# Expert stage of a fused attention and mixture-of-experts kernel: transposes move from TensorE to transposing DMAs on ScalarE's queue

## The chip, the cores and the metric

The kernel runs on one core of one Trainium2 chip. The metric is the device time of one execution in microseconds (us), the median of the runs shown. All rows come from one profiled execution of the same kernel.

## What is computed

The reference chains three stages. Only the last one, `_moe2_ref`, is touched here:

```
attn_out = _attn_ref(q, k, v, g_q, g_k)              # 4 x 12 heads, 448 x 64
x = attn_out as 1792 rows of 768
x = _moe_ref(x, w_gate, w_val, w_out)                # gated layer, 768 -> 1536 -> 768
# _moe2_ref: 8 experts, w1[e] is 768 x 1024, w2[e] is 1024 x 768
e_idx = argmax(x @ w_gate, axis=1)
gate_w = softmax(x @ w_gate) at e_idx
eom = sigmoid(x @ w_output_gate)
for e in range(8):
    mask = e_idx == e
    h = maximum(x[mask] @ w1[e], 0.0)
    ye = h @ w2[e]
    out[mask] = gate_w[mask, None] * eom[mask, e, None] * ye
```

Each row of x goes to one expert alone.

## The kernel before

Every matrix product of the fp32 data runs as three fp16 products: each operand is split into a high and a low fp16 part, and `PASSES` multiplies high by high, high by low and low by high. So a tile of 128 rows of x is 128 x 1536 fp16 (both parts), and a tile of the inner layer is 128 x 2048 fp16.

After the second stage the rows of x lie in DRAM as `y_parts`, high and low parts side by side. A routing table sorts them by expert into tiles of 128 rows, each tile of one expert. Tiles are numbered g from 0; an expert has one or more, and in this case there are 18. What each engine does for them is written out by hand as a function `tile(e, s, before, first)` for expert e, weight slot s, tile g = before + 1, and `over_experts` (line 381) calls it in loops whose bounds are read from the table. `first` marks an expert's first tile.

- **GpSimd** (`gather`, line 583) fetches the rows of tile g from `y_parts` into `x_rows`, two tiles ahead by its order but with one buffer only, so that it waits until the rows of the tile before have been transposed (`rows_turned`, line 601). `scatter` (line 606) stores finished rows.
- **TensorE** (`tile`, line 1533) does for tile g: `up` of half 0 (18 products of 128x512, line 1506), the transposes of the inner layer of the tile before (`turn_hidden`, 16 of 128x128, line 1515), `up` of half 1, the transposes of the gathered rows of tile g+1 (`turn_rows`, 12 of 128x128, line 1493), and `rows_down` of the tile before (48 products of 128x384, line 1528). Below, these are U0, U1 and D. `up` reads `x_t`, and `rows_down` reads `hid_t`; both are single buffers. Transposes land in PSUM.
- **VectorE** copies the transposed data from PSUM: `rows_out` (line 1229) into `x_t`, `turned_hidden` (line 1234) into `hid_t`. It also splits the inner layer (`hidden_split`, lines 1244 and 1246) and makes the low parts of the next expert's weights (`split_low`, line 1042).
- **ScalarE** (`tile`, line 838) takes the two halves of the inner layer out of PSUM with a Relu (line 848, hid0 and hid1 below), scales finished rows in `rows_done` (line 835, two instructions) once D has ended (`out_sum`), and makes the high parts of the next expert's weights (`split_high`, line 815). In an expert's first tile it makes three pieces before hid0, three between hid0 and hid1, and the last eight behind `rows_done`, so that these eight stand ahead of the next tile's hid0. Expert 1's first tile is an exception: there 14 pieces stand between hid0 and hid1 ("catch-up").
- **SyncE** loads the raw weights of the experts (line 512) into seven staging buffers, each as soon as `w_lo_ready` says that VectorE is done with it.

D of the tile before starts only when hid0 of the present tile is out, which also says that `rows_done` has emptied D's PSUM banks:

```
def tile(e, s, before, first):
    g = before + 1
    pe.wait_ge(x_t_ready, g + 1)
    up(e, s, g, 0, first)
    if not is_at(g, 0):
        turn_hidden(before, 0)
        turn_hidden(before, 1)
    up(e, s, g, 1, first)
    turn_rows(g + 1)
    if not is_at(g, 0):
        pe.wait_ge(hid_ready, 2 * g + 1)
```

Of the kernel before, what the change touches and what calls it, by code (L numbers as in the profile page):

```python
# [7 lines left out]
F16 = mybir.dt.float16  # L8
I32 = mybir.dt.int32
U32 = mybir.dt.uint32  # L10
ALU = mybir.AluOpType
# [45 lines left out]
def attention_moe_moe_kernel(nc, qk, v, v_last, g_qk, w_gate, w_val, w_out, w_out_t, router_w, out_gate_w,  # L57
# [19 lines left out]
    with ctx:  # L77
        def sem(name):
            return ctx.enter_context(nc.semaphore(name))
# [141 lines left out]
        hid = m2.take(128, F2, F32)  # L221
        hid_parts = m2.take(128, 2 * F2, F16).rearrange("p (l f) -> p l f", l=2)
        hid_t = m2.take(128, 2 * F2, F16).rearrange("p (b l c m) -> p b l c m", b=2, l=2, c=4)
# [104 lines left out]
        rows_turned = sem("rows_turned")  # L328
        x_t_ready = sem("x_t_ready")
# [4 lines left out]
        hid_turned = sem("hid_turned")  # L334
        hid_t_ready = sem("hid_t_ready")
        out_sum = sem("out_sum")
# [184 lines left out]
        def _(pool):  # L521
# [61 lines left out]
            def gather(g):  # L583

                if not isinstance(g, int):
                    read, turned, copied = pool.to_reg(16 * g), pool.to_reg(g), pool.to_reg(g + 1)
                    pool.wait_ge(route, ROUTE_DONE)
                    pool.wait_ge(gathered, read)
                else:
                    wait(pool, gathered, 16 * g)  # L590
                nc.gpsimd.tensor_copy(gather_idx, row_idx[:, bass.ds(g, 1)]).then_inc(gather_idx_ready, 1)
                if isinstance(g, int):
                    pool.wait_ge(gather_idx_ready, g + 1)
                    wait(pool, rows_turned, g)
# [56 lines left out]
        def _(act):  # L651
# [177 lines left out]

            def rows_done(g):  # L830

                act.wait_ge(out_sum, g + 1)
                act.wait_ge(scatter_idx_ready, g + 2)
                for b in range(2):
                    nc.scalar.activation(out_rows[:, b * HALF_DM:(b + 1) * HALF_DM], ps[:, 4 + b, 0:HALF_DM], ACT.Copy,  # L835
                                         scale=slot_w[:, bass.ds(g, 1)]).then_inc(out_ready, 1)

            def tile(e, s, before, first):
                g = before + 1
                more = first and not is_at(e, E - 1)  # L840
                if more and not is_at(g, 0):
                    act.wait_ge(hid_sum, 2 * g)
                    if not is_at(e, 1):
                        split_high(e + 1, 1 - s, range(0, KC // 2))
# [19 lines left out]
            rows_done(last_tile(act))  # L864

        @block.vector
        def _(dve):
# [354 lines left out]

            def rows_out(g):

                dve.wait_ge(rows_turned, g + 1)
                wait(dve, hid_sum, 2 * g)
                bank = 2 if is_at(g, 0) else 6
                for l in range(2):
                    last = nc.vector.tensor_copy(x_t[:, l].rearrange("p c m -> p (c m)"), ps[:, bank + l, :].bitcast(F16)[:, 0:DM])  # L1229
                last.then_inc(x_t_ready, 1)  # L1230
# [6 lines left out]
            rows_out(0)  # L1237
            split_low(0, 0, range(KC, PIECES))

            def hidden_split(g, b):  # L1240

                cols = slice(b * 512, (b + 1) * 512)
                dve.wait_ge(hid_ready, 2 * g + b + 1)
                nc.vector.tensor_copy(hid_parts[:, 0, cols], hid[:, cols]).then_inc(hid_hi_ready, 1)
                dve.wait_ge(hid_hi_ready, 2 * g + b + 1)
                nc.vector.tensor_tensor(hid_parts[:, 1, cols], hid[:, cols], hid_parts[:, 0, cols], ALU.subtract)\
                    .then_inc(hid_lo_ready, 1)

            def tile(e, s, before, first):
# [23 lines left out]
            over_experts(dve, tile)  # L1273
            last = last_tile(dve)
            turned_hidden(last, 0)
            turned_hidden(last, 1)

        @block.tensor
        def _(pe):
# [206 lines left out]

            def turn_rows(g):
                pe.wait_ge(gathered, 16 * g + 16)
                wait(pe, x_t_ready, g)
                bank = 2 if is_at(g, 0) else 6  # L1490
                for l in range(2):
                    for c in range(KC):
                        last = nc.tensor.transpose(ps[:, bank + l, :].bitcast(F16)[:, c * 128:(c + 1) * 128],  # L1493
                                                   x_rows[:, l * DM + c * 128:l * DM + (c + 1) * 128], ident)
                last.then_inc(rows_turned, 1)

            def up(e, s, g, b, first):


                if b == 1:  # L1500
                    wait(pe, hid_ready, 2 * g)
                for c in range(KC):
# [6 lines left out]

            def turn_hidden(g, b):  # L1510
                pe.wait_ge(hid_lo_ready, 2 * g + b + 1)
                for l in range(2):
                    for c in range(4):
                        at_c = b * 512 + c * 128
                        last = nc.tensor.transpose(ps[:, 2 + b, :].bitcast(F16)[:, (4 * l + c) * 128:(4 * l + c + 1) * 128],  # L1515
                                                   hid_parts[:, l, at_c:at_c + 128], ident)
                last.then_inc(hid_turned, 1)
# [31 lines left out]

            pe.wait_ge(route, ROUTE_DONE)  # L1550
            turn_rows(0)
# [47 lines left out]
```

## Time and profile before

| | |
|---|---|
| median of 3 runs | 1143.07 us (1142.74 to 1143.99) |
| the profiled execution's own time | 1139.88 us |
| its span | 1138.1 us |
| mean granted TensorE clock | 0.99 of full speed |
| TensorE busy | 1100.3 us, 97% of the span |
| VectorE busy | 594.7 us, 52% |
| ScalarE busy | 425.9 us, 37% |
| GpSimd busy | 256.5 us, 23% |
| first product of the expert stage | at 804.89 us of the span |

The span runs from the first to the last instruction of the profile. Busy time leaves out instructions that issue a DMA or wait. A share of DMA time is the mean over the core's 16 DMA engines. In a timeline each row is a run of like instructions with its start, its length and, in brackets, the idle time of that engine ahead of it with what ended it.

### The profile page before, as it was taken

The numbers are of one execution on the slowest core, as the hardware profiler recorded it, in microseconds if no ns is written. First come the engines' busy times: TensorE is split into PE (matmuls) and PEld (weight loads), VectorE is DVE, ScalarE is ACT, GpSimd is POOL, SyncE is SP. The second block draws the span as 40 slices with busy tenths as digits, with TensorE's granted clock in tenths as the row PEclk, the third lists the DMA queues.
The fourth block names the chain that finished last, engine by engine and source line by source line (L and its number), as shares of the span: only waits on it lengthen the run. The fifth ranks groups of instructions, "written<-read, shape, count | busy, mean of one in ns | idle before, by whom it ended". The sixth has DMA issues, their size and how long they took to land.

```text
span 1138.1 us, 17823 instructions
## 1 busy us (share of the span) xinstructions
PE 1100.3 (97%) x6617; PEld 573.3 (50%) x6618; DVE 594.7 (52%) x837; ACT 425.9 (37%) x631; POOL 256.5 (23%) x235
## 2 busy tenths in 40 slices
PE   7989999999999999999999999999898999999996
PEld 3434444444455555555555555556454555555554
DVE  7888888887433443333343300015656565556721
ACT  5768777777511111211111200001535253353510
POOL 4756767672200000000000000000211122112211
PEclk9999999999999999999999999999899999999999
DMA  5412222210121111111100501000848355366400
GB/s 144 122 49 62 61 65 58 66 25 17 60 67 56 56 55 55 55 55 55 55 28 1 195 28 41 28 32 23 296 163 319 118 211 206 108 217 225 142 20 18
DMA packets 71978, 104.11 MB, mean 91 GB/s; under 512 B 29310, under 2 KB 47870, under 8 KB 71920
## 3 DMA queue, kind: packets, MB, share of 16 engines
q1 hardware_dynamic: 63680, 89.84, 24.0%
q0 software_dynamic: 3120, 11.02, 2.7%
q10 hardware_dynamic: 5120, 2.48, 0.8%
q8 instruction: 36, 0.59, 0.2%
q14 instruction: 22, 0.18, 0.0%
HBM read 93.88 MB, written 13.76 MB: 95 GB/s over the span
## 4 chain that ended last, share of the span: by engine, by line
PE 87%; ACT 4%; DVE 4%; issue 2%; DMA 2%; ACTq 0%; POOL 0%; DVEq 0%; POOLq 0%; SPq 0%
PE ps L1434 29%; PE ps L1449 15%; PE ps L1528 12%; PE ps L1357 10%; PE ps L1506 7%; PE ps L1336 5%; PE ps L1316 2%; ACT arena L815 2%; DVE arena L1042 2%; PE ps L1348 2%; PE ps L1299 2%; PE ps L1338 1%; DMA arena<-in_moe_w 1%; PE ps L1515 1%; PE ps L1493 1%
## 5 line engine op out<-in xcount | busy, mean ns | idle before, releaser
L1434 PE MATMUL ps<-arena 128*128 128x448 f16 x1728 | 328.8, 352 | 0.0
L1434 PEld LDWEIGHTS ps<-arena 128*128 128x128 f16 x1728 | 168.1, 98 | 155.7
L1449 PE MATMUL ps<-arena 128*128 128x392 f16 (+1 forms) x1008 | 167.3, 329 | 2.4 <-DVE arena L1022 2.4
L1506 PE MATMUL ps<-arena 128*128 128x512 f16 x648 | 150.5, 388 | 5.6 <-DVE arena L1229 5.6
L1042 DVE SCALAR_TENSOR_TENSOR arena<-arena 128x768 f16<-128x768 f32 (+1 forms) x112 | 113.1, 1066 | 74.1 <-ACT arena L815 74.0
L1528 PE MATMUL ps<-arena 128*128 128x384 f16 x864 | 143.3, 326 | 4.0 <-DVE arena L1234 3.6
L1449 PEld LDWEIGHTS ps<-arena 128*128 (+1 forms) x1008 | 98.4, 98 | 70.4 <-DVE arena L1022 2.8
L1357 PE MATMUL ps<-arena 128*128 128x448 f32 x288 | 133.0, 573 | 0.0
L785 ACT ACTIVATE arena<-ps 128x448 f32<-128x448 f32 x48 | 26.1, 543 | 263.0 <-PE ps L1434 263.0
L1016 DVE SCALAR_TENSOR_TENSOR arena<-ps,arena 128x448 f32<-128x448 f32 x48 | 30.0, 624 | 176.0 <-PE ps L1434 96.1
L1528 PEld LDWEIGHTS ps<-arena 128*128 128x128 f16 x864 | 83.5, 98 | 58.6 <-issue 2.5
L940 DVE TENSOR_REDUCE arena<-ps 112x2 f16<-112x896 f32 x96 | 99.2, 1076 | 18.6 <-PE ps L1316 18.5
L815 ACT ACTIVATE arena<-arena 128x768 f16<-128x768 f32 (+1 forms) x112 | 97.5, 929 | 27.6 <-DMA arena<-in_moe_w 23.7
L1506 PEld LDWEIGHTS ps<-arena 128*128 128x128 f16 x648 | 63.7, 100 | 80.1 <-DVE arena L1229 6.4
L712 ACT ACTIVATE arena<-ps,arena 128x896 f32<-128x896 f32 x72 | 72.5, 1007 | 33.3 <-PE ps L1338 33.3
L960 DVE RECIPROCAL arena<-arena 128x448 f32<-128x448 f32 x24 | 70.8, 2951 | 10.3 <-ACT arena L730 10.3
L1336 PE MATMUL ps<-arena 64*128 64x448 f16 (+1 forms) x576 | 72.0, 356 | 3.0 <-ACT arena L712 1.7
L620 POOL MEMSET arena<- 128x1536 f16 x1 | 1.4, 1377 | 324.1 <-PE ps L1434 324.1
L835 ACT ACTIVATE arena<-ps,arena 128x384 f32<-128x384 f32 x36 | 18.9, 576 | 141.4 <-PE ps L1528 141.4
L1357 PEld LDWEIGHTS ps<-arena 128*128 128x128 f32 x288 | 47.6, 191 | 45.5 <-issue 45.5
L802 ACT ACTIVATE arena<-ps 128x768 f16<-128x768 f32 x14 | 11.3, 810 | 144.0 <-PE ps L1449 144.0
L1076 DVE TENSOR_SCALAR arena<-ps 128x16 f32 (+1 forms) x12 | 2.1, 171 | 119.9 <-ACT arena L802 119.9
(170 smaller groups left out, 1078.7 us busy)
## 6 DMA issues: line engine op xcount, KB each, us to landing
arena<-in_moe_w SPq DMA_DIRECT2D x48, 512.0 KB, 6.3
arena<-in_moe_w SPq DMA_DIRECT2D x64, 384.0 KB, 3.9
arena<-in_qk SPq DMA_DIRECT2D x23, 448.0 KB, 3.5
y_parts<-arena SPq DMA_DIRECT2D x16, 384.0 KB, 2.3
arena<-in_v SPq DMA_DIRECT2D x48, 96.0 KB, 2.6
arena<-in_moe_w_out SPq DMA_DIRECT2D x12, 384.0 KB, 5.5
arena<-in_w_out_t SPq DMA_DIRECT2D x11, 384.0 KB, 3.1
arena<-in_moe_w_gate SPq DMA_DIRECT2D x10, 384.0 KB, 4.2
```

The source lines that it names most:

```text
L712: nc.scalar.activation(probs[n % 2][:, :, i - 1], ps_pair(SCORE_SLOT, 128), ACT.Exp, bias=lift[:, 1:2])\
L815: nc.scalar.activation(hi, raw_rows(e, p), ACT.Copy, scale=S_OP).then_inc(w_hi_ready, 1)
L940: nc.vector.tensor_reduce(neg_max[n % 2][:, :, j], ps_pair(max_slot(n, j)), AX_X, ALU.max, negate=True)\
L960: nc.vector.reciprocal(sums_inv[n % 2], sums[n % 2]).then_inc(sums_inv_ready, 1)
L1016: nc.vector.scalar_tensor_tensor(gated[b % 2], ps[:, 2 * (b % 2) + 1, 0:S], 1.0 / S_OP, gate[b % 2], ALU.mult, ALU.mult).then_inc(gated_re ...
L1042: nc.vector.scalar_tensor_tensor(lo, raw_rows(e, p), S_OP, hi, ALU.mult, ALU.subtract).then_inc(w_lo_ready, 1)
L1336: nc.tensor.matmul(outs[h], qk_t[n % 3][rows, 1, kl, ks], qk_t[n % 3][rows, 0, ql], start=(kl + ql == 0), stop=False)
L1357: last = nc.tensor.matmul(ps[:, 6 + h, SQ], v_ones[n % 3][:, c, h * D:h * D + 2 * D], probs[n % 2][:, h, c], start=False, stop=(c == KCH - 1))
L1434: last = nc.tensor.matmul(ps[:, 2 * (b % 2) + g, 0:S], up_w[s][:, g, c, wl], xt[:, b * KC + c, xl], start=(c == 0 and wl + xl == 0), stop= ...
L1449: last = nc.tensor.matmul(ps[:, 4 + 2 * s + h, 0:cols], gt[:, f, gl, bass.ds(t * 128, 128)], wo[:, f, wl, h, 0:cols], start=(f == 0 and gl ...
L1506: last = nc.tensor.matmul(ps[:, b, :], x_t[:, xl, c], w1_s[s][:, c, wl, b * 512:(b + 1) * 512], start=(c == 0 and xl + wl == 0), stop=(c = ...
L1528: last = nc.tensor.matmul(ps[:, 4 + h, 0:HALF_DM], hid_t[:, b, hl, c], w2_s[s][:, k, wl, h * HALF_DM:(h + 1) * HALF_DM], start=(k == 0 and ...
```

## The change

`turn_rows` and `turn_hidden` leave TensorE, `rows_out` and `turned_hidden` leave VectorE. In their place ScalarE issues one transposing DMA for the rows of a tile (`x_rows` to `x_t`, 128 x 1536 fp16) and two for the halves of the inner layer (`hid_parts` to `hid_t`, 128 x 1024 fp16 each). Tile 0's rows are still transposed by TensorE. `hid_parts` changes its layout, so that a half lies in one piece, and VectorE's `hidden_split` waits until the half of the tile before has been transposed.

ScalarE issues the rows' DMA of tile g+1 behind hid1 of tile g. It issues the two DMAs of tile g's inner layer behind its wait for the end of D of tile g-1 (`out_sum`), since D reads `hid_t`, and ahead of the two copies of `rows_done`. For tile 0, which has no D ahead of it, they come directly behind the rows' DMA. The last tile's come in `rows_done` of the last call of `tile`. On ScalarE the names of the numbered lines are: 836 the rows' DMA, 844 the inner layer's, 858 the copies of `rows_done`, 871 the Relu, 816 `split_high`.

```diff
@@ gpsimd, gather
-                    pool.wait_ge(rows_turned, turned)
+                    pool.wait_ge(x_turned, turned)
@@ scalar
+            def turn_rows(g):
+
+                read = 16 * g + 16 if isinstance(g, int) else act.to_reg(16 * g + 16)
+                act.wait_ge(route, ROUTE_DONE)
+                act.wait_ge(gathered, read)
+                act.dma_start_transpose(x_t.rearrange("p l c m -> p (l c) m"), x_rows).then_inc(x_turned, 16)
+
+            def turn_hidden(g):
+
+                for b in range(2):
+                    split = 2 * g + b + 1 if isinstance(g, int) else act.to_reg(2 * g + b + 1)
+                    act.wait_ge(route, ROUTE_DONE)
+                    act.wait_ge(hid_lo_ready, split)
+                    act.dma_start_transpose(hid_t[:, b].rearrange("p l c m -> p (l c) m"), hid_parts[:, b].rearrange("p l f -> p (l f)"))\
+                        .then_inc(hid_turned[b], 16)
+
+            def rows_done(g, more_follow):
+
+                if more_follow:
+                    summed = act.to_reg(g + 1)
+                    act.wait_ge(route, ROUTE_DONE)
+                    act.wait_ge(out_sum, summed)
+                    turn_hidden(g + 1)
+                else:
+                    act.wait_ge(out_sum, g + 1)
...
+                turn_rows(g + 1)
                 if is_at(g, 0):
+                    turn_hidden(0)
                     split_high(e + 1, 1 - s, range(KC))
                 else:
-                    rows_done(before)
+                    rows_done(before, True)
@@ vector
-            def turned_hidden(g, b):
-                dve.wait_ge(hid_turned, 2 * g + b + 1)
-                nc.vector.tensor_copy(hid_t[:, b].rearrange("p l c m -> p (l c m)"), ps[:, 2 + b, :].bitcast(F16))\
-                    .then_inc(hid_t_ready, 1)
...
+                wait(dve, hid_turned[b], 16 * g)
+                nc.vector.tensor_copy(hid_parts[:, b, 0], hid[:, cols]).then_inc(hid_hi_ready, 1)
...
-                if not is_at(g, 0):
-                    turned_hidden(before, 0)
-                    turned_hidden(before, 1)
...
-                rows_out(g + 1)
@@ tensor
             def rows_down(e, s, g):
...
-                    pe.wait_ge(hid_t_ready, 2 * g + b + 1)
+                    pe.wait_ge(hid_turned[b], 16 * g + 16)
...
-                pe.wait_ge(x_t_ready, g + 1)
+                if is_at(g, 0):
+                    pe.wait_ge(first_x_ready, 1)
+                else:
+                    pe.wait_ge(x_turned, 16 * g)
                 up(e, s, g, 0, first)
-                if not is_at(g, 0):
-                    turn_hidden(before, 0)
-                    turn_hidden(before, 1)
                 up(e, s, g, 1, first)
-                turn_rows(g + 1)
...
-            turn_hidden(last, 0)
-            turn_hidden(last, 1)
```

TensorE before, one tile of the last expert (1506 is `up`, 1515 and 1493 the two kinds of transposes, 1528 `rows_down`):

```order
L1506 MATMUL ps<-arena 128x512 x18
L1511 ISA
L1515 MATMUL ps<-arena 128x128 x8
L1511 REGISTER_ALU
L1515 MATMUL ps<-arena 128x128 x8
L413 ISA
L1506 MATMUL ps<-arena 128x512 x18
L1488 ISA
L1493 MATMUL ps<-arena 128x128 x12
L1544 REGISTER_ALU
L1528 MATMUL ps<-arena 128x384 x48
```

TensorE with the change, the same tile (`up` is now line 1515, and 1523 is the wait for the turned inner layer):

```order
L413 ISA
L1515 MATMUL ps<-arena 128x512 x36
L1543 REGISTER_ALU
L1523 ISA
L1528 MATMUL ps<-arena 128x384 x48
```

The 28 transposes of a tile are gone, both halves of `up` run on without a break, and D of the tile before follows them at once.

ScalarE before, from hid1 of an expert's first tile to hid0 of the next tile, with what each instruction waits for:

```order
L848 ACTIVATE arena<-ps 128x512 [waits hid_lo_ready,hid_sum]
L833 REGISTER_ALU [waits out_sum]
L835 ISA [waits scatter_idx_ready]
L835 ACTIVATE arena<-ps,arena 128x384 x2
L815 ACTIVATE arena<-arena 128x768 [waits stage_loaded6]
L815 ACTIVATE arena<-arena 128x768 [waits stage_loaded0]
```

ScalarE with the change, the same place:

```order
L871 ACTIVATE arena<-ps 128x512 [waits hid_lo_ready,hid_sum]
L833 ISA
L836 DMA_TRANSPOSE arena<-arena 128x12x128 [waits gathered,route]
L844 DMA_TRANSPOSE arena<-arena 128x8x128 [waits route,hid_lo_ready,out_sum]
L844 DMA_TRANSPOSE arena<-arena 128x8x128 [waits hid_lo_ready,route]
L858 ISA [waits scatter_idx_ready]
L858 ACTIVATE arena<-ps,arena 128x384 x2
L816 ACTIVATE arena<-arena 128x768 [waits stage_loaded6]
L816 ACTIVATE arena<-arena 128x768 [waits stage_loaded0]
```

Three DMA issues now stand in ScalarE's order: one between hid1 and the wait for D's end, two between that wait and everything that follows it, the eight pieces of the weights and the next tile's hid0 among it.

## Rows read from the trace of the kernel before

**Rows 1.** The page's chain of work that ended last, by engine.

```profile
PE 87%; ACT 4%; DVE 4%; issue 2%; DMA 2%; ACTq 0%; POOL 0%; DVEq 0%; POOLq 0%; SPq 0%
```

**Rows 2.** Timeline of TensorE, tiles 4 to 7: start us, length us, what, idle before.

```profile
877.02 4.05 PE L1506 MATMUL ps<-arena 128*128 128x512 f16 x18
880.90 1.06 PE L1515 MATMUL ps<-arena 128*128 128x128 f16 x16
881.79 4.05 PE L1506 MATMUL ps<-arena 128*128 128x512 f16 x18
885.68 0.83 PE L1493 MATMUL ps<-arena 128*128 128x128 f16 x12
886.35 7.96 PE L1528 MATMUL ps<-arena 128*128 128x384 f16 x48
894.15 4.05 PE L1506 MATMUL ps<-arena 128*128 128x512 f16 x18
...
929.06 4.05 PE L1506 MATMUL ps<-arena 128*128 128x512 f16 x18
```

**Rows 3.** Timeline of ScalarE, tiles 5 and 6 (first and second of expert 2).

```profile
894.53 1.05 ACT L835 ACTIVATE arena<-ps,arena 128x384 f32<-128x384 f32 x2 [8.05 <-PE ps L1528]
896.23 2.95 ACT L815 ACTIVATE arena<-arena 128x1024 f16<-128x1024 f32 x3 [0.66 <-issue]
899.09 0.58 ACT L848 ACTIVATE arena<-ps 128x512 f32<-128x512 f32 x1
899.57 2.94 ACT L815 ACTIVATE arena<-arena 128x1024 f16<-128x1024 f32 x3
...
912.60 5.24 ACT L815 ACTIVATE arena<-arena 128x768 f16<-128x768 f32 x7
918.04 0.84 ACT L815 ACTIVATE arena<-arena 128x768 f16<-128x768 f32 x1 [0.21 <-DMA arena<-in_moe_w]
918.79 0.58 ACT L848 ACTIVATE arena<-ps 128x512 f32<-128x512 f32 x1
```

**Rows 4.** Timeline of TensorE, the first tiles of the stage.

```profile
816.56 0.84 PE L1493 MATMUL ps<-arena 128*128 128x128 f16 x12 [2.04 <-DMA arena<-y_parts,arena]
818.52 5.75 PE L1506 MATMUL ps<-arena 128*128 128x512 f16 x18 [1.12 <-DVE arena L1229]
...
837.35 4.05 PE L1506 MATMUL ps<-arena 128*128 128x512 f16 x18
...
857.00 5.56 PE L1506 MATMUL ps<-arena 128*128 128x512 f16 x18 [2.36 <-DVE arena L1229]
```

**Rows 5.** Timeline of ScalarE, catch-up of expert 1: its first piece and the hid1 behind its last.

```profile
841.93 5.23 ACT L815 ACTIVATE arena<-arena 128x768 f16<-128x768 f32 x7
...
858.57 0.58 ACT L848 ACTIVATE arena<-ps 128x512 f32<-128x512 f32 x1
```

**Rows 6.** Timeline of TensorE, the last tile.

```profile
1120.09 1.06 PE L1515 MATMUL ps<-arena 128*128 128x128 f16 x16
1121.57 7.97 PE L1528 MATMUL ps<-arena 128*128 128x384 f16 x48 [0.43 <-ACT arena L835]
```

**Rows 7.** Timeline of ScalarE in the first stage: DMAs issued from its own queue.

```profile
27.12 0.39 ACTq L676 DMA_DIRECT2D arena<-in_moe_w_gate  x1
...
29.15 2.01 ACTq L676 DMA_DIRECT2D arena<-in_moe_w_val  x1
```

**Rows 8.** DMA issues: engine, count, KB each, median us from issue to landing.

```profile
arena<-in_moe_w SPq DMA_DIRECT2D x48, 512.0 KB, 6.3
...
y_parts<-arena SPq DMA_DIRECT2D x16, 384.0 KB, 2.3
...
arena<-in_moe_w_gate ACTq DMA_DIRECT2D x1, 24.0 KB, 3.1
```

**Rows 9.** Landing of the gathers (line 602, 384 KB each), least, median and most.

```profile
DMA to landing us min/median/max: 2.2/5.8/7.8
```

**Rows 10.** DMA queue of ScalarE: packets, MB, share of the 16 engines' span.

```profile
q10 hardware_dynamic: 5120, 2.48, 0.8%
```

**Rows 11.** Windows of 4 us in tiles 5 and 6: engines' busy time, clock, DMA share, GB/s.

```profile
904.00:908.00 4.00, 4.00 (x26) 2.42 (x25) 3.97 (x7) 0.00 (x0) 2.06 (x2) 1.00 0.57 175
...
920.00:924.00 4.00, 3.52 (x30) 2.29 (x29) 3.97 (x8) 0.60 (x1) 1.25 (x2) 1.00 1.00 404
```

More of the change, by code:

```diff
@@ L221, in attention_moe_moe_kernel @@
         hid = m2.take(128, F2, F32)
-        hid_parts = m2.take(128, 2 * F2, F16).rearrange("p (l f) -> p l f", l=2)
+        hid_parts = m2.take(128, 2 * F2, F16).rearrange("p (b l f) -> p b l f", b=2, l=2)
         hid_t = m2.take(128, 2 * F2, F16).rearrange("p (b l c m) -> p b l c m", b=2, l=2, c=4)
@@ L328, in attention_moe_moe_kernel @@
         rows_turned = sem("rows_turned")
-        x_t_ready = sem("x_t_ready")
+        first_x_ready = sem("first_x_ready")
+        x_turned = sem("x_turned")
         hid_sum = sem("hid_sum")
@@ L333, in attention_moe_moe_kernel @@
         hid_lo_ready = sem("hid_lo_ready")
-        hid_turned = sem("hid_turned")
-        hid_t_ready = sem("hid_t_ready")
+        hid_turned = [sem(f"hid_turned{b}") for b in range(2)]
         out_sum = sem("out_sum")
@@ L585, in gather @@
                 if not isinstance(g, int):
-                    read, turned, copied = pool.to_reg(16 * g), pool.to_reg(g), pool.to_reg(g + 1)
+                    read, turned, copied = pool.to_reg(16 * g), pool.to_reg(16 * g - 16), pool.to_reg(g + 1)
                     pool.wait_ge(route, ROUTE_DONE)
@@ L593, in gather @@
                     pool.wait_ge(gather_idx_ready, g + 1)
-                    wait(pool, rows_turned, g)
+                    wait(pool, rows_turned, min(g, 1))
+                    wait(pool, x_turned, 16 * (g - 1))
                     if is_at(g, 0):
@@ L828, in _ @@
             split_high(0, 0, range(KC, PIECES))
-            def rows_done(g):
-                act.wait_ge(out_sum, g + 1)
+            def turn_rows(g):
[18 more added lines that the diff above has]
+                    act.wait_ge(out_sum, g + 1)
                 act.wait_ge(scatter_idx_ready, g + 2)
@@ L863, in _ @@
             over_experts(act, tile)
-            rows_done(last_tile(act))
+            rows_done(last_tile(act), False)
         @block.vector
@@ L1221, in _, with first_rows_out @@
             y_low(TT - 1, 1)
[L1223 to L1227, printed above, removed]
+            def first_rows_out():
+                dve.wait_ge(rows_turned, 1)
                 for l in range(2):
-                    last = nc.vector.tensor_copy(x_t[:, l].rearrange("p c m -> p (c m)"), ps[:, bank + l, :].bitcast(F16)[:, 0:DM])
-                last.then_inc(x_t_ready, 1)
-            def turned_hidden(g, b):
-                dve.wait_ge(hid_turned, 2 * g + b + 1)
-                nc.vector.tensor_copy(hid_t[:, b].rearrange("p l c m -> p (l c m)"), ps[:, 2 + b, :].bitcast(F16))\
-                    .then_inc(hid_t_ready, 1)
-            rows_out(0)
+                    last = nc.vector.tensor_copy(x_t[:, l].rearrange("p c m -> p (c m)"), ps[:, 2 + l, :].bitcast(F16)[:, 0:DM])
+                last.then_inc(first_x_ready, 1)
+            first_rows_out()
             split_low(0, 0, range(KC, PIECES))
@@ L1243, in hidden_split @@
                 dve.wait_ge(hid_ready, 2 * g + b + 1)
-                nc.vector.tensor_copy(hid_parts[:, 0, cols], hid[:, cols]).then_inc(hid_hi_ready, 1)
+                wait(dve, hid_turned[b], 16 * g)
+                nc.vector.tensor_copy(hid_parts[:, b, 0], hid[:, cols]).then_inc(hid_hi_ready, 1)
                 dve.wait_ge(hid_hi_ready, 2 * g + b + 1)
-                nc.vector.tensor_tensor(hid_parts[:, 1, cols], hid[:, cols], hid_parts[:, 0, cols], ALU.subtract)\
+                nc.vector.tensor_tensor(hid_parts[:, b, 1], hid[:, cols], hid_parts[:, b, 0], ALU.subtract)\
                     .then_inc(hid_lo_ready, 1)
@@ L1273, in _ @@
             over_experts(dve, tile)
-            last = last_tile(dve)
-            turned_hidden(last, 0)
-            turned_hidden(last, 1)
         @block.tensor
@@ L1484, in _, with turn_first_rows @@
             down(TT - 1, 1, range(4, FC))
[L1487 to L1490, printed above, removed]
+            def turn_first_rows():
+                pe.wait_ge(gathered, 16)
                 for l in range(2):
                     for c in range(KC):
-                        last = nc.tensor.transpose(ps[:, bank + l, :].bitcast(F16)[:, c * 128:(c + 1) * 128],
+                        last = nc.tensor.transpose(ps[:, 2 + l, :].bitcast(F16)[:, c * 128:(c + 1) * 128],
                                                    x_rows[:, l * DM + c * 128:l * DM + (c + 1) * 128], ident)
@@ L1497, in up @@
             def up(e, s, g, b, first):
-                if b == 1:
-                    wait(pe, hid_ready, 2 * g)
+                wait(pe, hid_ready, 2 * g + b - 1)
                 for c in range(KC):
@@ L1508, in up @@
                 last.then_inc(hid_sum, 1)
[L1510 to L1517, printed above, removed]
             def rows_down(e, s, g):
@@ L1550, in _ @@
             pe.wait_ge(route, ROUTE_DONE)
-            turn_rows(0)
+            turn_first_rows()
             over_experts(pe, tile)
             last = last_tile(pe)
-            turn_hidden(last, 0)
-            turn_hidden(last, 1)
             pe.wait_ge(out_ready, 2 * last)
```

## The prediction

> **What bounds the kernel now.** I read the chain of waits by engine first: 87% of it is TensorE [rows 1], so time leaves this kernel only where TensorE stops working or waiting. Then TensorE's timeline in the stage touched. A tile is five pieces on end without a gap: U0, transposes of the inner layer, U1, transposes of the rows, D. From 877.02 to 894.15 that is 17.13 us [rows 2]. The differences of the starts give U0 3.88, inner transposes 0.89, U1 3.89, row transposes 0.67, D 7.80. Products alone are 15.57, so the two kinds of transposes cost 1.56 us a tile. Third, ScalarE's timeline, because the change puts its DMAs there. In an expert's first tile and at the head of its second ScalarE is nearly full: the row copies, 3 + 3 pieces of weights around hid0, later eight more [rows 3]. Where these eight stand ahead of hid0, hid0 starts at 918.79 and D could start at 919.4; TensorE was ready for D only at 920.6. ScalarE has 1.2 us to spare there, and the change takes TensorE's work away and adds to ScalarE's.
>
> **What goes.** At most 1.56 us x 18 tiles = 28.1 us of TensorE, plus short waits of D for VectorE's copy. VectorE's copies vanish too, which is worth nothing by itself.
>
> **What comes: two unknown prices.** The trace has no transposing DMA. (a) The time for which ScalarE's queue is held by one issue, C. A plain issue with 768 pieces took 0.39 us when the queue was empty and 2.01 us as the fourth in a row [rows 7]. A transposing DMA has 1024 or 1536 pieces of 256 bytes if it is read so, and the two for the inner layer follow each other. I take 2.0 for each, the row with the queue filled, and keep 0.4 as the lower end. (b) The time L from its issue to its landing. A plain store of 384 KB out of the same memory takes 2.3 us, weight loads with several in flight take 6.3 [rows 8], gathers of 384 KB take 2.2 to 7.8, median 5.8 [rows 9]. The DMA share in tiles 5 and 6 is 0.57 to 1.00 [rows 11], so I take 7.0 for the rows (issue included) and 5.5 for half an inner layer.
>
> The Trainium skill, "Advanced Engine Details and Errata", section "X-Bar Transpose (TRN2)", holds that a transposing DMA is as fast as a plain one; no row here shows one. By that, L would lie near the 2.3 us of the plain store where the DMA engines are free, and the sum would be that of rival A.
>
> **The sum.** Let T be the end of a D, on which ScalarE waits.
>
> *Plain tiles* (4, 9, 16, 17). hid1 is done 7.77 + 0.6 after T, so the rows land at T + 8.4 + 7.0 = 15.4, just before D of the tile ends at 15.57. The inner layer lands at T + 7.5, before the next D at T + 7.77. So 1.56 us saved each: 4 x -1.56 = -6.2.
>
> *First and second tile of experts 2 to 6* (5 pairs; one takes 929.06 - 894.15 = 34.91 now [rows 2]). First tile: two issues 4.0, copies 1.05, gap and three pieces 3.60 (895.58 to 899.18), hid0 0.49 [rows 3], together 9.14. D waits for it: it runs from T + 9.14 to 16.94, where it could have begun at 7.77. Then three pieces (2.84) and hid1 (0.6) end at 12.6, and the rows land at 19.6. TensorE stands idle from 16.94 to 19.6. Second tile: ScalarE starts at 16.94: 4.0, copies 1.05, gap 0.1, eight pieces with their wait 6.3 (912.60 to 918.88), hid0 0.5, so D may start at 28.9; TensorE is ready at 19.6 + 7.77 = 27.4. D ends at 36.7. The pair takes 36.7 for 34.9: +1.8, five times +9.0. What is late next is the weights' pieces behind the two issues, but they have the rest of the tile.
>
> *The start.* Tile 1's rows land in x_rows at 816.56, and U0 starts at 818.52 behind TensorE's 0.84 and VectorE's copy [rows 4]. There is no D to cover the DMA, so U0 starts at 816.56 + 7.0 = 823.6. U0 5.6 and U1 3.9 follow, D ends at 840.9, where it was 837.35 [rows 4]: +3.6. ScalarE then issues two more (4.0) and copies, so hid0 of tile 2 ends at 846.5. Here the catch-up starts, which ran from 841.93 to 858.57 [rows 5], partly waiting for loads. Before, VectorE copied tile 3's rows in the middle of it, and U0 of tile 3 could start at 857.00. Now ScalarE issues that DMA behind the whole catch-up: starts 4.6 later, some of its waits for loads vanish, I put its end at 861 and hid1's at 861.6. The rows land at 868.6, U0 starts 11.6 us later than before. With 5.5 + 3.9 for the two halves and 7.8 for D, tile 4 starts at 885.8 against 877.02: +8.8.
>
> *The end.* The last tile's inner layer may only be transposed when the D before it has ended. Now 1.48 us lie between that and the last D (1120.09 to 1121.57 [rows 6]); with the change it is 5.5: +4.0. The second half's landing is covered by the first half of D.
>
> Together 8.8 + 9.0 - 6.2 + 4.0 = +15.6. The profiled execution took 1139.88, so 1155.5; the median of the runs is 3.2 above that execution, so 1158.7, say **1159 us**. With the bounds left open around it this case reaches from 1146 to 1210.
>
> **Rival A: the DMA is cheap.** C = 0.5, L = 4.0. First tile: hid0 at T + 6.1, D not delayed, rows landed at 13.6: 15.57. Second: D may start at 9.0, ends at 16.8. A pair is 32.3 instead of 34.9: five times -2.6 = -13.0. Plain -6.2. Start: rows at 820.6, end of D at 837.9, hid1 of the catch-up at 859.6, rows of tile 3 at 863.6, tile 4 starts +3.8. End: +1.5. Sum -13.9: 1126 for the execution, **1129** as a median. For it speak the 2.3 us of the plain store; against it the pieces of 256 bytes, and the bursts of weight loads that fall on just these tiles. The point that decides is C: every us on it adds 2 us to each hid0 that stands behind the two issues. At C = 1.2 and L = 6 the sum is about nil.
>
> **Rival B: the DMA engines (or the issue itself) become the bound.** Each tile turns 12 + 8 + 8 blocks of 128x128. ScalarE's queue moved 5120 packets in 0.8% of 16 engines' span, 28 ns each [rows 10]. If only the reads count, 3584 pieces of 256 bytes on 16 engines are 6.4 us a tile, hidden. If every 32-byte run that is written costs as much, that is 28,672 pieces or 51 us a tile, and 18 x (51 - 17) = +610. That small pieces are dear is to be seen in 24 KB that took 3.1 us, more than 384 KB in long ones [rows 8]. A price of 18 us a tile, near the geometric middle, and 7 us of weight loads (6.3 MB an expert at 404 GB/s [rows 11], 8 experts on 18 tiles) make 25 us instead of 17.1: **about 1285**. That the two patterns spread over fewer than 16 engines would look the same.
>
> The Trainium skill, "VectorE: DVE Perf Modes", section "The three transpose paths", gives 1309 ns for a 128x128 fp16-sized block by DMA and 390 ns by TensorE. As an estimate from that page, 28 blocks one after the other would be 36.7 us, and the time near 1490. TensorE's own block here goes by faster than the page's figure: 0.89 us for 16, that is 56 ns [rows 2].
>
> **How the numbers follow.** The forecast (issue and landing of middling price) 0.47, rival A 0.29, rival B 0.24. A measurement of this kernel can tell about 0.2% (2.3 us) from no change. Faster than 1140.8: 0.26, nearly all of A. Within: 0.07, the seam between A and the forecast. Slower: 0.67. The range reaches from 1122 (A with L at 2.3 to 3) to 1340, which takes in the nearer half of B; about 0.05 lie below and 0.13 above.
>
> **What the next profile would show.** ScalarE's queue rows for the transposing DMAs, with their length (2.0?) and landing (7 and 5.5?). TensorE's tile in plain stretches: 15.6 us, with no row of 128x128 products but tile 0's. Idle time ahead of U0, released by the rows' DMA: some 5 us at tile 1, most at tile 3, 2.7 in second tiles. Idle time ahead of D released by ScalarE's copies or Relu in the pairs, 1.4 to 1.5 us each. About 5.5 us ahead of the last D. I am wrong if the landing of the rows is under 4 us and the issue under 0.6 (then A), or if TensorE waits in plain tiles too, by 8 us or more (then B).

## The result and the profile after

The changed kernel takes 1186.58 us (median of 4, 1182.73 to 1193.4) against 1142.9 us of the kernel before beside it: a ratio of 1.039, with a 95% interval of 1.034 to 1.044. It is slower, as forecast, but by 43.7 us where 15.6 were forecast. Its profiled execution has a span of 1183.5 us, 45.4 more than before.

The page of the changed kernel, engines' busy time, then queues, then the chain of waits by engine:

```profile
PE 1090.2 (92%) x6113; PEld 547.8 (46%) x6114; DVE 557.1 (47%) x765; ACT 424.8 (36%) x631; POOL 252.1 (21%) x235
...
q1 hardware_dynamic: 63680, 89.84, 24.6%
q10 hardware_dynamic: 71360, 19.01, 10.0%
...
PE 76%; DMA 11%; ACT 3%; ACTq 3%; issue 3%; DVE 2%; POOL 1%; POOLq 0%; SPq 0%; DVEq 0%
```

TensorE is busy for 10.1 us less and idle for 55.5 us more. The chain that was TensorE's for 87% [rows 1] is TensorE's for 76%, and 11% of it is DMA. ScalarE's queue moved 66,240 packets more [rows 10]. Its share rose by 9.2 points of the time of the 16 DMA engines (16 x 1183.5 us), so 26 ns a packet, and 6.05 us of all 16 engines for each of the 18 tiles.

Who waited for whom on TensorE from 800 us on, total, times, longest:

```profile
PE ps L1515 <- DMA arena<-arena: 51.2, 12, 17.6
PE ps L1528 <- ACT arena L871: 5.0, 4, 3.0
PE ps L1528 <- ACT arena L858: 4.1, 1, 4.1
PE ps L1528 <- DVE arena L1067: 3.5, 3, 2.5
```

Here 1515 is `up` and 1528 is D. Most of the idle time stands ahead of U0, and the rows' DMA ends it. TensorE's timeline shows where (U0 and U1 are one row of 36 products now):

```profile
825.28 10.81 PE L1515 MATMUL ps<-arena 128*128 128x512 f16 x36 [9.77 <-DMA arena<-arena]
...
877.05 10.52 PE L1515 MATMUL ps<-arena 128*128 128x512 f16 x36 [17.59 <-DMA arena<-arena]
...
897.83 7.94 PE L1515 MATMUL ps<-arena 128*128 128x512 f16 x36 [2.45 <-DMA arena<-arena]
...
913.40 7.93 PE L1515 MATMUL ps<-arena 128*128 128x512 f16 x36
922.05 7.97 PE L1528 MATMUL ps<-arena 128*128 128x384 f16 x48 [0.71 <-ACT arena L871]
935.06 10.53 PE L1515 MATMUL ps<-arena 128*128 128x512 f16 x36 [5.03 <-DMA arena<-arena]
946.12 7.97 PE L1528 MATMUL ps<-arena 128*128 128x384 f16 x48 [0.53 <-ACT arena L871]
957.40 9.62 PE L1515 MATMUL ps<-arena 128*128 128x512 f16 x36 [3.31 <-DMA arena<-arena]
...
1122.39 7.97 PE L1528 MATMUL ps<-arena 128*128 128x384 f16 x48 [2.97 <-ACT arena L871]
1130.20 7.93 PE L1515 MATMUL ps<-arena 128*128 128x512 f16 x36
1137.97 7.96 PE L1528 MATMUL ps<-arena 128*128 128x384 f16 x48
1145.77 7.93 PE L1515 MATMUL ps<-arena 128*128 128x512 f16 x36
...
1165.56 9.65 PE L1528 MATMUL ps<-arena 128*128 128x384 f16 x48 [4.05 <-ACT arena L858]
```

Tile 4 starts at 897.83 instead of 877.02 [rows 2]; 1.0 us of that lies ahead of the stage. The pair of tiles 5 and 6 takes 957.40 - 913.40 = 44.0 us instead of 34.9. Tiles 16 and 17, beside which no weights are loaded, run as the forecast's plain tiles do: 15.57 us from one U0 to the next. A row of 36 products takes 7.93 us, but 9.6 to 10.8 behind most of the longer waits. From tile 1 on there are twelve waits of 2 us or more, and behind ten of them the next row of products is 1.7 to 2.9 us longer. Behind two it is not: 2.45 us ahead of tile 4, and 2.97 us ahead of the D at 1122.39.

ScalarE's queue, in its timeline: a DMA's issue with its length, first beside weight loads, then in the quiet tiles (the second row is the copies of `rows_done`).

```profile
866.60 9.62 ACTq L844 DMA_TRANSPOSE arena<-arena  x2
879.14 1.05 ACT L858 ACTIVATE arena<-ps,arena 128x384 f32<-128x384 f32 x2 [13.51 <-POOL arena L612]
...
921.52 2.29 ACTq L836 DMA_TRANSPOSE arena<-arena  x1
...
930.42 7.67 ACTq L844 DMA_TRANSPOSE arena<-arena  x2
...
1138.32 1.29 ACTq L836 DMA_TRANSPOSE arena<-arena  x1
1146.02 2.64 ACTq L844 DMA_TRANSPOSE arena<-arena  x2
```

And the 18 DMAs of the rows (line 836), least, median and most:

```profile
L836 ACTq DMA_TRANSPOSE arena<-arena x18: 1290/1924/6012, 818.5 to 1153.9; - x18
...
DMA to landing us min/median/max: 3.7/9.6/13.4
```

The DMA at 1138.32, which sees no weight loads, holds the queue for 1.29 us and lands in 3.7. The median one lands in 9.6, the worst in 13.4. In the five pairs nine of the ten land in 8.1 to 13.4 us.

Late rows hold up more than TensorE. GpSimd fetches the next rows only when these have been transposed, and behind that it writes the scatter index (line 612) for which ScalarE's copies wait. At tile 3 the two issues ended at 876.22, the rows landed at 876.93, and the copies began only at 879.14.

Two windows of the changed kernel, while loads and a transposing DMA were both in flight, with the columns of [rows 11]:

```profile
925.40:929.40 4.00, 4.00 (x27) 2.39 (x26) 3.17 (x4) 0.00 (x0) 0.00 (x0) 1.00 1.29 102
...
933.40:937.40 4.00, 2.34 (x6) 0.89 (x7) 0.00 (x0) 0.00 (x0) 1.25 (x2) 0.51 1.03 327
```

In the first the DMA engines are taken all the time (packets on one engine overlap, so the share passes 1.00) and move 102 GB/s, where loads alone move 404 in such a window [rows 11]. In the second, which holds the end of a wait of 5.03 us and the first products behind it, TensorE's granted clock is 0.51, its lower level of 1.2 GHz.

### The profile page after: what moved, and what is told of

Same layout as the page of the kernel before. It is cut to its first block, busy times and chain, and to the rows that moved or that the text cites. A ratio compares the mean times of both kernels' runs of the same rounds, so it can differ in the third digit from the quotient of the medians.

```text
span 1183.5 us, 16771 instructions
## 1 busy us (share of the span) xinstructions
PE 1090.2 (92%) x6113; PEld 547.8 (46%) x6114; DVE 557.1 (47%) x765; ACT 424.8 (36%) x631; POOL 252.1 (21%) x235
## 4 chain that ended last, share of the span: by engine, by line
PE 76%; DMA 11%; ACT 3%; ACTq 3%; issue 3%; DVE 2%; POOL 1%; POOLq 0%; SPq 0%; DVEq 0%
PE ps L1446 28%; PE ps L1461 14%; PE ps L1369 10%; DMA arena<-arena 8%; PE ps L1515 6%; PE ps L1528 6%; PE ps L1348 4%; PE ps L1328 2%; DMA arena<-in_moe_w 2%; ACTq L844 2%; PE ps L1311 2%; PE ps L1360 1%; PE ps L1350 1%; ACT arena L816 1%; DVE arena L1067 1%
## 5 line engine op out<-in xcount | busy, mean ns | idle before, releaser
L1446 PEld LDWEIGHTS ps<-arena 128*128 128x128 f16 x1728 | 168.1, 98 | 155.7
L1515 PE MATMUL ps<-arena 128*128 128x512 f16 x648 | 161.0, 413 | 53.4 <-DMA arena<-arena 51.2
L1528 PE MATMUL ps<-arena 128*128 128x384 f16 x864 | 146.8, 331 | 12.6 <-ACT arena L871 5.0
L1515 PEld LDWEIGHTS ps<-arena 128*128 128x128 f16 x648 | 66.9, 105 | 144.6 <-issue 80.0
L1528 PEld LDWEIGHTS ps<-arena 128*128 128x128 f16 x864 | 84.8, 99 | 74.9 <-issue 16.1
L816 ACT ACTIVATE arena<-arena 128x768 f16<-128x768 f32 (+1 forms) x112 | 97.0, 928 | 33.4 <-DMA arena<-in_moe_w 19.8
L603 POOL DMA_INDIRECT arena<-y_parts,arena x20 | 21.8, 1090 | 220.3 <-DMA arena<-arena 219.3
```

The costliest lines, as they stand in the source:

```text
L816: nc.scalar.activation(hi, raw_rows(e, p), ACT.Copy, scale=S_OP).then_inc(w_hi_ready, 1)
L1446: last = nc.tensor.matmul(ps[:, 2 * (b % 2) + g, 0:S], up_w[s][:, g, c, wl], xt[:, b * KC + c, xl], start=(c == 0 and wl + xl == 0), stop= ...
L1515: last = nc.tensor.matmul(ps[:, b, :], x_t[:, xl, c], w1_s[s][:, c, wl, b * 512:(b + 1) * 512], start=(c == 0 and xl + wl == 0), stop=(c = ...
L1528: last = nc.tensor.matmul(ps[:, 4 + h, 0:HALF_DM], hid_t[:, b, hl, c], w2_s[s][:, k, wl, h * HALF_DM:(h + 1) * HALF_DM], start=(k == 0 and ...
```

## The experiments

After the result there were three suspects: the landing beside weight loads (Q), the hold of ScalarE's queue by the issues (I) and its order (O), and TensorE's clock behind waits (K). Of each edit the lines that matter are shown; `...` marks a gap.

**One kind of transposes each.** rows_only keeps `turn_hidden` on TensorE and `turned_hidden` on VectorE; hid_only keeps `turn_rows` and `rows_out` there.

```diff
--- rows_only, from the changed kernel
-                    turn_hidden(g + 1)
...
--- hid_only, from the changed kernel
-                turn_rows(g + 1)
...
```

> Only the gathered rows are transposed by DMA; the inner layer goes through TensorE and VectorE as before. Theory Q (a transposing DMA lands late while weight loads share the DMA engines, and the rows' DMA has only one D, 7.8 us, to hide behind): nearly the whole loss is here. 40 to 51 us of TensorE waiting ahead of U0 and some 8 us of slower clock, less 18 x 0.67 saved: 1170 to 1185 us. Theory I (each issue holds ScalarE's queue for 1.3 to 6 us, and the pieces of weights and hid0 behind it come late): the rows' issue stands where ScalarE waits for D anyway, so little is lost but at tiles 1 and 3: 1145 to 1155 us.

> Only the inner layer is transposed by DMA; the rows go through TensorE and VectorE as before. Theory Q: its landing has U0 and U1 to hide behind, and the first half may be late by up to 1 us: saved 18 x 0.89 = 16 us, lost 2.5 us at the end and about 1 us a pair in ScalarE's delay: 1130 to 1140 us. Theory I: 36 of the 54 issues are here, 2.6 to 9.6 us a tile ahead of the row copies, the eight pieces and hid0: D waits for hid0 in every pair: 1155 to 1175 us.

Measured: rows_only 1163.91 us, ratio 1.017 (1.014 to 1.019); hid_only 1157.82 us, ratio 1.012 (1.010 to 1.014). Neither theory has both. The rows cost 20 us, below Q's range and above I's; the inner layer costs 14 us, in I's range. Waits on TensorE in rows_only, where 1515 is `up` and 1537 D, with the landing of its 18 DMAs:

```profile
PE ps L1515 <- DMA arena<-arena: 34.3, 7, 17.3
PE ps L1537 <- DVE arena L1247: 8.9, 6, 2.8
...
DMA to landing us min/median/max: 3.6/6.0/12.6
```

and in hid_only, where 1523 is D, with the landing of its 36 DMAs:

```profile
PE ps L1523 <- ACT arena L862: 11.0, 3, 4.7
PE ps L1523 <- DVE arena L1057: 7.9, 3, 2.7
...
DMA to landing us min/median/max: 3.1/3.3/8.4
```

So the two halves of the change lose in different ways. The rows' DMA lands late, and U0 waits for it. The inner layer's lands in 3.3 us and is in time, but D waits for ScalarE and VectorE, which come late behind the issue.

The two losses add to 34 us, not 44, and the traces show where the rest arises. From the stage's first product to the start of tile 4 rows_only is 21.0 us behind the kernel before, hid_only 6.1, the changed kernel 19.8. From there to the start of the last D it is 4.1, 8.3 and 23.2. So behind tile 4 the two halves are dearer together. In rows_only the rows that are issued in the pairs' first tiles land in 5.2 to 7.2 us, where the changed kernel has 8.1 to 13.4. In tile 5 one sees why: in rows_only the DMA's packets fall into a gap of the loads (926 to 929 us, 45 of the loads' packets in three us), while in the changed kernel it is issued at 921.52, just as the loads start, and its packets run among theirs. For the other pairs this was not looked at packet by packet.

**The order at the catch-up.**

```diff
-                        if is_at(e, 1):
-                            split_high(e, s, range(KC, PIECES))
-                            split_high(e + 1, 1 - s, range(0, KC // 2))
...
                 turn_rows(g + 1)
+                if more and is_at(e, 1):
+                    split_high(e, s, range(KC, PIECES))
+                    split_high(e + 1, 1 - s, range(0, KC))
```

> The changed kernel, but in expert 1's first tile ScalarE takes hid1 and issues the rows' DMA ahead of the 14 pieces of the catch-up instead of behind them. The changed kernel waits 17.6 us ahead of tile 3 for these rows. If the order on ScalarE is the cause of that wait (Q and I both say so), it shrinks to the 5 us that other tiles wait or to what the late weights leave, 1172 to 1180 us. If the loads of the weights bound this stretch anyway, the wait moves to the next D or U0: 1184 to 1188 us.

Measured: 1183.09 us (1172.53 to 1189.12), ratio 1.036 (1.032 to 1.039), not to be told from the changed kernel's 1.039, and in neither expected range. The profiled execution is the fastest of the four, 1172.53 us; the other three took 1183 to 1189. Waits of its TensorE:

```profile
PE ps L1515 <- DMA arena<-arena: 24.6, 9, 11.6
PE ps L1528 <- ACT arena L871: 18.2, 4, 14.2
```

The 17.6 us ahead of U0 of tile 3 are gone, and 14.2 us stand ahead of the D behind it instead, where the pieces now delay hid0. The order sets the place of that wait. What moving it gains can't be told: nothing by the median, while the one profiled execution lies inside the range expected for a gain.

**The clock.**

```diff
                 g = before + 1
+                if not is_at(g, 0) and not is_at(e, E - 1):
+                    keep_busy()                            # 10 products of 128x512 into an unused bank
```

> The changed kernel with ten more products of 128x512 (2.2 us at full clock, results unused) ahead of each tile's wait for its rows, in experts 0 to 6. Theory K (a part of the loss is that TensorE's clock falls to its lower level after a wait and U0 then runs 1.7 to 2.6 us longer): where the wait is over 2.2 us the products cost nothing and U0 and U1 go back from 9.6 to 7.9 us: 8 to 9 waits, 10 to 15 us less, but about 2.2 us more at each of the 4 tiles that wait for nothing: 1172 to 1182 us. If the clock plays no part: 1186 to 1200 us.

Measured: 1177.84 us, ratio 1.030 (1.027 to 1.033), 8.7 us below the changed kernel, although ten products were added to each of 15 tiles, tiles that had no wait among them. Three rows of its timeline, the added products (line 1535) and the `up` behind them:

```profile
952.59 2.32 PE L1535 MATMUL ps<-arena 128*128 128x512 f16 x10
956.80 7.94 PE L1515 MATMUL ps<-arena 128*128 128x512 f16 x36 [1.89 <-DMA arena<-arena]
...
1049.05 7.94 PE L1515 MATMUL ps<-arena 128*128 128x512 f16 x36 [0.45 <-DMA arena<-arena]
```

These are tiles 7 and 12, which took 9.62 and 9.63 us in the changed kernel behind waits of 3.31 and 2.23. From tile 1 on `up` takes 138.0 us in all instead of 151.4, so K holds as a part of the loss. At tiles 1 and 3 the wait outlasts the ten products (9.09 and 14.45 us more), and there U0 and U1 still take 9.57 and 9.32 us.

**Fewer bytes of weights, and more.**

```diff
--- light_before, light_after
-                    sp.dma_start(raw_rows(e, p), piece(e, s, p)[0]).then_inc(stage_loaded[p % STAGES], 16)
+                    few = (F2 if p < KC else DM) // (1 if isinstance(e, int) else 4)
+                    sp.dma_start(raw_rows(e, p)[:, 0:few], piece(e, s, p)[0][:, 0:few]).then_inc(stage_loaded[p % STAGES], 16)
--- endload_before, endload_after
+            sp.wait_ge(w_lo_ready, PIECES * E)
+            for k in range(24):
+                wait(sp, more_loaded[k % STAGES], 16 * (k // STAGES))
+                sp.dma_start(stage[k % STAGES], w1_d[k % 8, 0]).then_inc(more_loaded[k % STAGES], 16)
```

> The kernel before, with only the first quarter of the columns of each weight piece loaded for experts 2 to 7 (the same number of loads, a quarter of the bytes; the stale rest is split as if it were weights). All theories: before waits for loads only around tiles 2 to 4, so 1138 to 1143 us.

> The changed kernel with the same quarter loads. Theory Q (traffic: transposing DMAs land late because weight loads are on the DMA engines with them): landing of the rows goes back to about 3.7 us in nearly every tile, the waits ahead of U0 vanish from tile 5 on, and what is left is the start (10 to 20 us more than before up to tile 4), about nil in the pairs and 4 to 6 us at the end, less 1.56 us in plain tiles: 1150 to 1162 us. Theory O (order: ScalarE's issues and the catch-up are late by themselves, whatever the loads): 1175 to 1185 us as with full loads.

> The kernel before, with 24 more loads of 512 KB, not used by anything, once the last weights are split, so that the last two tiles, which saw no loads, now run beside them. Before has nothing there but gathers and scatters on the DMA engines, which it can wait for: within 2 us of before, 1141 to 1146 us.

> The changed kernel with the same 24 loads behind its last weights. In the changed kernel tiles 16 and 17 wait for nothing and their DMAs land in 3.7 and 3.3 us. Theory Q: beside full loads the rows land in 10 to 13 us, so that U0 of tile 17 waits 3 to 6 us, the inner layer's first half comes late, and the end waits 8 to 12 us instead of 4: 1195 to 1210 us. Theory O: 1186 to 1190 us.

Measured: light_before 1140.42 us, ratio 0.997 (0.995 to 0.998); light_after 1149.27 us, ratio 1.005 (1.003 to 1.006). The change costs 8.9 us beside quarter loads and 43.7 beside full ones. The expectation's range for light_after, 1150 to 1162, was just missed on the low side. Its waits (1516 is `up`, 1529 D) and the landing of its rows' DMAs:

```profile
PE ps L1529 <- ACT arena L872: 18.2, 11, 3.1
PE ps L1516 <- DMA arena<-arena: 13.7, 2, 9.7
...
DMA to landing us min/median/max: 3.7/4.3/6.5
```

From tile 4 on U0 waits for nothing. What remains are the start, D's waits for hid0 and the end.

endload_before took 1143.43 us, ratio 1.000 (0.999 to 1.001); endload_after 1201.41 us, ratio 1.052 (1.047 to 1.056), 14.8 us above the changed kernel, in the range of Q. The place was another than expected: not U0 of tile 17 but D ahead of it, behind an issue that held ScalarE's queue for 11.23 us. ScalarE's queue, TensorE and a window of endload_after (851 is the inner layer's DMA, 1535 D):

```profile
1127.90 11.23 ACTq L851 DMA_TRANSPOSE arena<-arena  x2
...
1143.32 6.47 PE L1535 MATMUL ps<-arena 128*128 128x384 f16 x24 [7.74 <-DMA arena<-arena]
1154.48 5.76 PE L1535 MATMUL ps<-arena 128*128 128x384 f16 x24 [4.69 <-DMA arena<-arena]
...
1134.00:1138.00 4.00, 1.59 (x8) 0.50 (x6) 0.00 (x0) 0.00 (x0) 0.00 (x0) 1.00 1.04 404
```

In the changed kernel this tile waited for nothing and its pair of issues took 3.4 us. The edit adds nothing but these loads, 404 GB/s in this window. With both edits, fewer bytes and more, the landing follows the traffic. So Q holds: it is the traffic beside them that makes the transposing DMAs late.

**The issue by itself.** In the kernel before, two transposing DMAs that nobody uses.

```diff
                 else:
+                    if more:
+                        hold(e, before)
                     rows_done(before)
...
+            def hold(e, before):
...
+                act.wait_ge(out_sum, summed)
...
+                for b in range(2):
+                    src = at_slot[:, b * 512:b * 512 + 1024]
+                    dst = early_stage[1].bitcast(F16)[:, b * 1024:(b + 1) * 1024]
+                    act.dma_start_transpose(dst.rearrange("p (c m) -> p c m", c=8), src).then_inc(held, 16)
```

> The kernel before, whole, plus two transposing DMAs of 128x1024 fp16 between parts of the buffers that nothing reads any more, issued by ScalarE in the first tiles of experts 1 to 6 at the place where the changed kernel issues the inner layer's: behind the wait for the end of D, ahead of the row copies and the eight pieces. Nobody waits for their landing. It prices the issue alone. Before, hid0 of the next tile is done 1.2 us ahead of TensorE and D starts 0.48 us later still. With 2.65 us of issue hid0 is 1.45 us late, so D starts 0.8 to 1.5 us later in each of 6 tiles: 1148 to 1153 us, and D is released by ScalarE's Relu there. If an issue costs ScalarE nothing that matters: 1143 to 1145 us.

Measured: 1166.5 us (1160.19 to 1169.82), ratio 1.019 (1.016 to 1.021): six pairs of issues cost 22 us, where 4 to 9 were expected. The profiled execution is the slowest of the five, 1169.82 us. ScalarE, VectorE and TensorE of this kernel in tile 6 (841 the DMAs, 861 hid0 and hid1, 1058 VectorE's low pieces, 1250 its copy of the turned inner layer, 1544 D):

```profile
921.85 2.65 ACTq L841 DMA_TRANSPOSE arena<-arena  x2
924.72 1.05 ACT L848 ACTIVATE arena<-ps,arena 128x384 f32<-128x384 f32 x2 [10.79 <-issue]
925.66 6.21 ACT L816 ACTIVATE arena<-arena 128x768 f16<-128x768 f32 x8
...
926.53 7.04 DVE L1058 SCALAR_TENSOR_TENSOR arena<-arena 128x768 f16<-128x768 f32 x8 [7.73 <-ACT arena L816]
933.49 1.28 DVE L1250 COPY arena<-ps 128x1024 f16<-128x1024 f16 x2
...
934.32 9.64 PE L1544 MATMUL ps<-arena 128*128 128x384 f16 x48 [3.22 <-DVE arena L1250]
```

The expectation counted ScalarE's 1.2 us to spare. But VectorE makes eight low pieces behind ScalarE's eight high ones and copies the inner layer after them, and D had been waiting 0.48 us for that copy all along. There was nothing to spare: the whole 2.65 us goes to D (3.22 us of wait for 0.48), and D then takes 9.64 us for 7.97 at the lower clock, 4.4 us for this pair. All five pairs behind the catch-up wait 3.2 us; the longer D follows in four of them (9.3 to 9.6 us), and in the fifth D takes 7.96. At the catch-up D waits 7.75 us where it waited 1.21, but there the issues are not alone: ScalarE's pieces wait 2.93 us for a load, 1.43 before. In tile 6 the eight pieces take 6.21 us where they took 6.28 [rows 3], so there it is the issue and not slower loads.

**A version built on this.** From the kernel before: DMAs for the inner layer only where no eight pieces of weights stand behind the issue. All rows stay on TensorE.

```diff
+        def by_dma(e, nth):
+
+            return is_at(nth, 0) == is_at(e, E - 1)        # nth: place of the tile in its expert
...
+                    if turn:
+                        turn_hidden(g + 1)
```

> From the kernel before. The inner layer is transposed by DMA only where the trace of hid_only showed nothing waiting for it: for tiles that are not an expert's first in experts 0 to 6, and for expert 7's first, 10 of 18 (1, 3, 4, 6, 8, 9, 11, 13, 15, 16). There no eight pieces of weights stand behind the two issues. All other inner layers, the last tile's among them, and all rows stay on TensorE. It holds where every expert has at least two tiles, as here. If the issue's hold of 2.65 us ahead of the eight pieces was what cost hid_only its gain, 10 x 0.89 = 8.9 us are saved and no D waits longer than before: 1133 to 1138 us, a ratio of 0.992 to 0.996. If the DMAs hurt in themselves (slower weight loads, landing in a burst), 1143 us or more.

Measured: 1138.13 us (1136.34 to 1139.94), ratio 0.995 (0.993 to 0.996): 6.5 us faster than the kernel before and 48 us faster than the changed one, at the upper end of what was expected. From the start of tile 4 to the last D it takes 238.5 us where the kernel before takes 244.6: 6.0 of the 8.0 us that the nine inner layers turned by DMA there could save. Up to tile 4 it is not faster: at the catch-up D waits 2.55 us, where it waited 1.21. It needs at least two tiles for every expert.

## Why the prediction was wrong

**The sign and its reason held.** TensorE's 1.56 us a tile are saved, in plain tiles exactly: 15.57 us from one U0 to the next in tiles 16 and 17. The throughput of the DMA engines was not the bound either: 6.05 us of them a tile, where the working for rival B had 6.4 us if only reads of 256 bytes counted.

By the parts of the sum, up to the end of the last D, with the 1.0 us ahead of the stage left out:

| part | forecast | measured |
|---|---|---|
| start, up to tile 4 | +8.8 | +19.8 |
| five pairs | +9.0 | +25.0 (174.5 to 199.5) |
| tiles 4 and 9 | -3.1 | -1.4 |
| tiles 16, 17 and the end | +0.9 | +1.3 |
| sum | +15.6 | +44.7 |

**Two steps failed: the price of the landing and the clock.**

The first is L = 7.0 us for the landing of the rows. It was one number for all tiles, and the trace has two: 3.7 to 4.1 us where no weights are loaded, and 8.1 to 13.4 in the pairs beside loads. The row that it leaned on, loads with several in flight (6.3 us [rows 8]), shows plain DMAs beside plain DMAs. It says nothing of small pieces beside large ones. light_after shows the size: with L at 4.3 in the median nothing waits ahead of U0 in the pairs, five of them take 179.8 us in place of 199.5, and the change as a whole costs 8.9 us.

The second is the clock behind the waits, put at nothing. The forecast carried it only where [rows 4] show it, in U0 of tiles 1 and 3 (5.6 and 5.5 us for 3.9), and not behind the waits that it forecast itself: 2.7 us in every second tile and 5.5 at the end. From tile 1 on the rows of `up` and D are together 19.9 us longer than 7.93 and 7.96 us each, against 3.2 in the trace before. The experiment on it, warm10, gave 8.7 us of the whole time back.

The five pairs, taken apart by the differences of the starts, over the 31.14 us of products in each:

| in five pairs | forecast | measured |
|---|---|---|
| waits ahead of U0 | 13.3 | 22.9 |
| waits ahead of D | 14.4 | 9.9 |
| lower clock | 0 | 11.1 |
| sum (rounded) | 27.7 | 43.8 |

So of the 16 us that the pairs missed, the waits of U0 are 9.6 and the clock is 11.1; D's waits, forecast too long, took 4.5 off. The two belong together: with less waiting there is less of the lower clock, 11.6 us in light_after where the changed kernel has 19.9.

**C was mis-sized the other way in quiet tiles.** An issue takes 1.25 to 1.5 us there, once 2.6, not 2.0. Beside loads it can be far longer: of the 18 pairs five took 4.4 to 9.6 us, the others 2.6 to 3.7, and four issues of rows took 5.6 to 6.0. The chain from the issue over the eight pieces to hid0 was right in kind: in light_after D of the second tiles waits 2.7 to 3.1 us, where 2.65 + 1.05 + 0.1 + 6.3 + 0.5 - 7.77 = 2.8. The 1.2 us that ScalarE was said to have to spare in the kernel before were not there: D waited for VectorE's copy behind the pieces, as hold shows.

**The start.** The first wait was right: the gather landed at 818.4 and U0 started 6.9 us later, at 825.28. Tile 3's U0 then started 7.4 us later than forecast: 3.0 because the catch-up ended later (hid1 from 865.05 to 865.63), 4.4 by the landing, 12.5 us after the issue. The clock added 1.0 to U0 and U1 of tile 3 beyond the forecast, and a wait ahead of tile 4, which was not forecast, 2.6.

**The end** came near: 4.05 us of wait instead of 5.5, and then 1.7 us for the clock.

**The rivals.** A's price was that of a quiet chip, and light_after comes nearest to it, and it is still 8.9 us slower than light_before. B's mechanism is half there: the engines are taken for 100% of the time at 102 GB/s in some windows of a burst, but not over a tile. The rule of the Trainium skill, "Advanced Engine Details and Errata", section "X-Bar Transpose (TRN2)", that these DMAs are as fast as plain ones, does not hold here: 384 KB take 3.7 us where a plain store of as much to DRAM takes 2.3 [rows 8], and 9.6 in the median over all tiles. The 1309 ns a block of the Trainium skill, "VectorE: DVE Perf Modes", section "The three transpose paths", do not add up over one DMA either: 12 blocks land in 3.7 us.

What is not settled is why the two kinds of traffic slow each other so. endload_after has the loads at their full 404 GB/s while the transposing DMAs starve: in its window 413 of their packets are in flight, 18 ns each. The changed kernel has windows in which both crawl: at 925.40 the loads and the transposing DMA move some 51 GB/s each, and a transposing DMA's packet takes 69 ns in the mean, 18 in the median, so some stand very long. No run separates the size of the pieces from the transposing itself; plain DMAs with pieces of 256 bytes beside the loads would. Nor was a second buffer for `x_rows` or `x_t` tried, with which the rows could be issued earlier.

## What to carry to other kernels

A transfer that is hidden in a quiet trace is not hidden in a burst: price its landing from the traffic that will be beside it, not from the median of others. To give it more than one stage to hide behind is what this suggests; no run here tried it. An issue on a compute engine's queue is work of that engine; before it is put ahead of something, look not only at that engine's spare time but at who paces itself by it. A wait of 2 us or more on TensorE cost 1.7 to 2.9 us again in the clock behind it in ten of twelve cases here, so it belongs in the sum. What moved badly as a whole may still pay in the places where nothing stands behind it, as in mixed.

## What was not expected of the hardware

- A transposing DMA holds ScalarE's queue for 1.25 to 1.5 us beside no loads (once 2.6), over three times the 0.39 us of a plain one issued first [rows 7], and two in a row held it for 11.2 us beside full loads.
- Beside loads at about 400 GB/s its landing goes from 3.7 to as much as 18.7 us in endload_after, while the gathers of the kernel before, which also run beside loads, stay within 7.8 us [rows 9].
- With both in flight the 16 engines were fully taken and moved 102 GB/s.
- Its packets are of 256 bytes: 66,240 packets for 54 DMAs and 16.5 MB, 32 of 4 bytes in each DMA among them.
- The length of a wait alone does not say whether TensorE's clock is lower behind it. In light_after D takes 9.65, 9.36 and 9.65 us behind waits of 3.06, 2.91 and 2.72 us, and 7.97 behind waits of 2.72 and 2.91.
